# The last eight blocks of an expert layer in nested branches, with a change of w2 and the last down product taken by halves

## What is computed

```python
def _moe2_ref(x, modality_id, w_gate, modality_bias, w1, w2):
    N, D = x.shape                      # 3072 tokens, 384; 8 experts; w1: 384 x 1024, w2: 1024 x 384 each
    logits = x @ w_gate + modality_bias[modality_id]
    e_idx = np.argmax(logits, axis=1)
    ...
    gate_w = probs[np.arange(N), e_idx]
    for e in range(E):
        mask = e_idx == e
        if not mask.any():
            continue
        h = np.maximum(x[mask] @ w1[e], 0.0)
        out[mask] = gate_w[mask, None] * (h @ w2[e])
```

## Time and profile before

| | us |
|---|---|
| median of 3 runs | 916.67 (913.45 to 918.15) |
| the profiled execution | 912.8 |
| its span, first to last instruction | 911.1 |
| PE busy with matmuls | 835.3 (92% of the span) |
| mean granted clock of TensorE | 0.968 |

### The profile page before, as it was taken

The page is one execution under the profiler, slowest core; times in us unless marked ns, Lnnn a source line. Parts: engine busy times, 40 slices in busy tenths (PEclk is TensorE's granted clock), DMA queues, the critical chain, the costliest instruction groups (busy, mean ns, idle before and its releaser), DMA issues.

```text
span 911.1 us, 26166 instructions
## 1 busy us (share of the span) xinstructions
PE 835.3 (92%) x10528; PEld 740.3 (81%) x10529; DVE 567.3 (62%) x1598; ACT 351.0 (39%) x613; POOL 86.4 (9%) x100
## 2 busy tenths in 40 slices
PE   3674699999999999999999999999989999999993
PEld 3564588889888888888888888789868999999993
DVE  5958896888677877787688843344743333333342
ACT  4463246443644454345533432424412222222231
POOL 1000000000010000100010000010121222212211
PEclk9977699999999999999999999999999999999997
DMA  8942453256226541484134313246151111111104
GB/s 120 306 110 46 85 136 80 65 110 135 48 55 111 119 72 29 101 147 72 29 90 99 71 44 80 56 85 204 35 174 45 43 44 35 51 36 43 43 19 148
DMA packets 148679, 77.94 MB, mean 86 GB/s; under 512 B 112864, under 2 KB 144608, under 8 KB 148192
## 3 DMA queue, kind: packets, MB, share of 16 engines
q1 hardware_dynamic: 143632, 66.59, 33.1%
q0 software_dynamic: 4096, 9.48, 3.4%
q10 hardware_dynamic: 848, 0.39, 0.2%
HBM read 59.30 MB, written 13.21 MB: 80 GB/s over the span
## 4 chain that ended last, share of the span: by engine, by line
PE 79%; DVE 5%; ACT 5%; DMA 3%; SPq 3%; issue 3%; ACTq 1%; POOL 0%; DVEq 0%; POOLq 0%
PE bank L560 21%; PE bank L541 19%; PE bank L627 11%; PE bank L652 10%; PE bank L637 2%; ACT gram_d L1081 2%; PE bank L442 2%; PE bank L462 2%; PE bank L411 1%; PE bank L522 1%; PE bank L490 1%; PE bank L422 1%; PE bank L473 1%; PE bank L398 1%; DMA kq_in_rows<-in_k 1%
## 5 line engine op out<-in xcount | busy, mean ns | idle before, releaser
L560 PE MATMUL bank<-wo_hi,g_hi 128*128 128x392 f32 x384 | 135.6, 353 | 1.9 <-DVE g_lo L1536 1.9
L560 PE MATMUL bank<-wo_lo,g_hi 128*128 128x392 f32 x384 | 131.1, 341 | 0.0
L560 PE MATMUL bank<-wo_hi,g_lo 128*128 128x392 f32 x384 | 130.8, 341 | 0.0
L541 PE MATMUL bank<-x_hi,wi_hi 128*128 128x512 f32 x288 | 119.9, 416 | 11.3 <-DVE x_lo L1527 10.6
L1154 ACT ACTIVATE g_raw<-bank 128x512 f32<-128x512 f32 x96 | 57.4, 598 | 169.6 <-PE bank L541 169.4
L1531 DVE SCALAR_TENSOR_TENSOR g_raw<-g_raw 128x512 f32<-128x512 f32 x96 | 66.1, 688 | 81.8 <-ACT g_raw L1154 81.2
L541 PE MATMUL bank<-x_hi,wi_lo 128*128 128x512 f32 x288 | 114.5, 397 | 0.0
L541 PE MATMUL bank<-x_lo,wi_hi 128*128 128x512 f32 x288 | 114.4, 397 | 0.0
L1161 ACT ACTIVATE g_hi<-g_raw 128x512 fp32r<-128x512 f32 x96 | 60.8, 633 | 98.9 <-DVE g_raw L1531 98.9
L1536 DVE TENSOR_TENSOR g_lo<-g_raw,g_hi 128x512 fp32r<-128x512 f32 x96 | 66.1, 689 | 30.9 <-ACT g_hi L1161 29.6
L560 PEld LDWEIGHTS bank<-wo_hi,g_hi 128*128 128x128 f32 x384 | 72.3, 188 | 7.1 <-issue 3.1
(11 more groups left out here) (215 smaller groups left out, 1451.3 us busy)
## 6 DMA issues: line engine op xcount, KB each, us to landing
wo_lo<-wo_lo_d SPq DMA_DIRECT2D x80, 196.0 KB, 2.6
w_raw<-in_moe_w SPq DMA_DIRECT2D x4, 1536.0 KB, 7.8
x_rows<-stage SPq DMA_DIRECT2D x24, 192.5 KB
kq_in_rows<-in_k SPq DMA_DIRECT2D x6, 768.0 KB, 7.0
k_raw<-in_k SPq DMA_DIRECT2D x24, 192.0 KB, 4.1
vals<-in_v SPq DMA_DIRECT2D x48, 96.0 KB, 2.7
kq_in_rows<-in_q SPq DMA_DIRECT2D x6, 768.0 KB, 7.0
x_raw<-y_t SPq DMA_DIRECT2D x33, 96.0 KB, 2.5
```

What stands on the lines that cost most here:

```text
L541: mm = pe.matmul(bank[0][:], a[:, m, P * f:P * f + P], x[:, m, :], start=(m == 0 and x is x_hi and a is wi_hi), stop=(m == KT - 1 and a is ...
L560: mm = pe.matmul(acc[i][:, 0:DX], g[f % 2][:, P * i:P * i + P], w, start=(f == 0 and k == 0), stop=(f == FT - 1 and k == 2))
```

## The change

Three things are changed.

1. Blocks 23 to 30 are written out, each in the branch of the block before, with no loop. Their table loads have fixed addresses. When block 25 has no tokens, one jump leads behind all of it.
2. In `act_block` and `dve_block`, for all blocks from 2 on, the second half of a new w2 is made behind `split_ht`, and on DVE behind `gated` too, not ahead of them. The decision is loaded once and branched on twice.
3. The down product that comes by itself behind the last block waits by halves: for the first half of `w_lo` and `ht_lo`, then 12 matmuls, then for the second half, then 12 matmuls.

```diff
-            def block_down(x, count=None):
+            def block_down(x, count=None, by_halves=False):
...
-                pe.wait_ge(w2l[0], count)
-                pe.wait_ge(w2l[1], count)
-                pe.wait_ge(s.ht_rdy, b * 2 + 2)
+                if not by_halves:
+                    pe.wait_ge(w2l[0], count)
+                    pe.wait_ge(w2l[1], count)
+                    pe.wait_ge(s.ht_rdy, b * 2 + 2)
                 for h in range(2):
+                    if by_halves:
+                        pe.wait_ge(w2l[h], count)
+                        pe.wait_ge(s.ht_rdy, b * 2 + h + 1)
...
-            with pe.Fori((TOKT - 1) // 2, (BLOCKS - 1) // 2) as i:
-                with pe.If(has_tokens(pe, Blk(i, 1)) > 0):
-                    pe_block(Blk(i, 1))
-                    with pe.If(first_without(pe, Blk(i, 2)) > 0):
-                        block_down(Blk(i, 1))
-                    with pe.If(has_tokens(pe, Blk(i, 2)) > 0):
-                        pe_block(Blk(i, 2))
-                        with pe.If(first_without(pe, Blk(i, 3)) > 0):
-                            block_down(Blk(i, 2))
+            def last_blocks(x):
+                pe_block(x)
+                with pe.If(first_without(pe, x.next()) > 0):
+                    block_down(x, by_halves=True)
+                if x.n < BLOCKS - 1:
+                    with pe.If(has_tokens(pe, x.next()) > 0):
+                        last_blocks(x.next())
+
+            last_blocks(Blk(0, TOKT - 1))
...
             def act_block(x):
...
-                with act.If(changes(act, x) > 0):
-                    change_w2(x)
+                change = changes(act, x)
+                with act.If(change > 0):
+                    change_w2(x, 0)
                 split_ht(x.n)
+                with act.If(change > 0):
+                    change_w2(x, 1)
...
             def dve_block(x, kept=False):
...
-                with dve.If(changes(dve, x) > 0):
-                    change_w2(x)
+                change = changes(dve, x)
+                with dve.If(change > 0):
+                    split_w2(0, expert_count(dve, x))
                 gated(x.next(-1))
                 split_ht(x.n)
+                with dve.If(change > 0):
+                    split_w2(1, expert_count(dve, x))
```

## The result

| | us |
|---|---|
| before, median of 7 runs | 913.76 (912.04 to 918.15) |
| changed, median of 7 runs | 909.73 (907.89 to 910.92) |
| ratio changed to before | 0.9935, 95% interval 0.9919 to 0.9951 |
| profiled execution of the changed kernel | 909.23, its span 907.4 |

The ratio is 5.9 us of 913.76 (4.5 to 7.4). The difference of the two medians is 4.0 us and that of the two means 5.2, so the size of the gain is uncertain by some 1.5 us. I had forecast 3.1. The direction was right and the size was not; the time lies nearest to rival (a). It is 3.9 us under the 913.6 that I named, but 2.9 of that is the kernel of before, whose median came out at 913.76 here and at 916.67 in the three runs that I added my forecast to. So the gain is what is to be compared, and not the time.

What follows compares the result with a forecast made beforehand. It took the kernel to be bound by PE's matmuls (79% of the span). With `o_sb` 3.7 us earlier but the drain starting at the landing, it gained 3.1 us: 916.67 - 3.1 = 913.6 us, range 909.0 to 918.5.

Steps and rivals of the forecast that it cites:

- rival (a): At the end, POOL's drain runs beside the transfers: gain 5.7 us, 911.0, or 912.4 with the lower clock; chance 0.32.
- The chain in block 24: Last down product: PE's gap shrinks from 4.2 to 1.9 us, a 0.25 us wait inside, `o_sb` 3.7 us earlier.
- The clock: PE's clock stays at its upper level in the last down product, giving 1.4 of the 3.7 us.
- The empty turns: At the end, POOL's three empty loop turns go, so its drain is reached at most 2.0 us earlier.
- The landing: Block 24's scatter, started at 897.9, lands at 901.5, just behind the load of w2.
- The drain: At the end, POOL's 6.3 us drain starts only when the last scatter lands: end at 908.0, gain 3.1 us.
- (b): Last scatter held up by the load, taking 7.4 us to land: 917.4 us; chance 0.18 together with smaller losses.
- (c): At the end, the jump over six blocks costs POOL 2.1 us of code fetch: 913.1 us; chance 0.07.
- (d): Blocks 3 to 22: one more branch on ACT and DVE holds up the sequencer: slower, 923.6 us; chance 0.05.

Runs made afterwards that it cites:

- e6: The changed kernel, with POOL waiting until its last scatter has landed before it goes to the drain; ratio to before 0.9975.
- e0: The kernel of before, unchanged, profiled once more in one execution; 912.54 us.
- e3: The changed kernel, with its last down product waiting for everything at once as before; ratio to before 0.9988.
- e2: The kernel of before with its loop, with w2 and ht by halves and the last down product waiting by halves; ratio to before 0.9955.
- e7: The changed kernel without the scatter of block 24 and without the unused loads behind the last expert; ratio to before 0.9860.
- e5: The changed kernel without the unused loads of w1 and w2 behind the last expert; ratio to before 0.9917, 908.11 us.

## Why the prediction was right and wrong, step by step

**The chain in block 24: right.** I said a gap of 1.9 us, a stop of 0.25 in the middle, and `o_sb` 3.7 us earlier from the last turning; measured 1.70, 0.16 (0.05 ahead of the 13th matmul and 0.11 behind it) and 3.84. **The clock: right, by a choice that no row settled.** It stayed at 1.00 throughout; ahead of the last product it fell with gaps of 3.7 to 4.3 us in every profile, and with 1.7 to 1.8 in none. In between it goes either way: behind block 4's gather PE stood for 2.4 to 2.6 us, and the clock fell to 0.50 in the changed kernel and 0.54 in e6, but not in e0 and e3. It also fell behind the broken stretch of the earlier trace rows, so a short gap alone is no guarantee.

**The empty turns: right in kind, 1.5 us and not 2.0.** I let the drain begin at the end of the scatter instruction, with 6.3 us; it takes 6.3 to 6.45 us from there, a little more than the 6.28 of a POOL that comes late.

**The landing: 0.7 us short, and without consequence.** I put it at 901.5 for a scatter started at 897.9, 3.6 us; it took 4.3. It did come when I said, just behind the load of w2 (903.7 and 903.5).

**The drain: wrong, and this step carries nearly the whole error.** "I take the first reading of the drain, by a little ... no row decides it." The sum let the 6.3 us begin at the landing, 901.5, and not at 898.9, where POOL is through with its scatter; those 2.6 us were never spent. The trace held one fact, that 6.28 us passed with the scatter landed, and both readings fit it. The changed kernel, e2 and e6 decide for the other one: the drain is over 3.1 us behind the landing, takes its 6277 ns with the scatter in flight, and waiting for the landing first adds the wait in full (13.0 us behind `o_sb`, not 9.5). By rival (a) the sum was 5.7 us; the profiles show 5.4 and the runs 5.9 (the profiles' sum is 3.8 from the chain, where I had 3.7, and 1.5 from the turns, where I had 2.0). The Trainium skill, page "VectorE: DVE Perf Modes", section "The DRAIN you can't avoid", puts the drains that the runtime adds at a program's beginning and end at a constant of about 12 ns on all engines. The drain here stands in the kernel's own closing barrier, and the traces don't tell whether the section would count it; POOL's is 6.19 to 6.94 us in eleven profiles, and the measurement decides.

**The rivals.** (a) came true, at the upper clock. (b), a late landing, could not matter. (c), the fetched code, is real as a stall (that it is a fetch is argued only), and mostly larger than I priced it (2.6 to 6.6 us against 2.1), but falls on the engines that POOL covers, and not on POOL. (d), the extra branch in blocks 3 to 22, costs nothing. The turning of h in block 3 and that in block 24 stand 21 blocks apart; the first of them in the changed kernel:

```profile
691.11 1.03 PE L637 MATMUL bank<-ident,h_sb 128*128 128x128 f32 x8
```

From there to 890.59 it is 199.5 us; in the kernel of before the same stretch ran from 689.16 to 888.93, 199.8 us.

**The chances.** I gave no clear change 0.57 and faster by over 0.5% only 0.36, and it came out faster by 0.65%. The two readings of the drain lay on either side of that bound, and I had leaned to the wrong one.

## What to carry over

Read the end of a program backwards from its last instruction: here 6.3 of the 22 us behind the last block's turning were the drain of one engine, and 2.0 more its empty turns ahead of it, so what counts is when that engine is through with its last transfer instruction and at its drain. When halves are taken in turn, move both sides at once: the producer's order without the consumer's wait, or the wait without the order, gained nothing at `o_sb`. And when one measured duration allows two readings that price a change differently by 2.6 us, the forecast is as uncertain as the choice between them.

## What the runs showed of the hardware that I had not expected

- POOL's drain in the closing barrier ended 6.2 to 6.45 us behind the end of its last indirect transfer's instruction, or behind POOL's arrival where that was later, landed or not, and with the last transfer left out too. POOL's 2.0 us of empty turns before it took nothing off (6.28 us in before, e0 and e2).
- A taken branch over the code of six blocks held PE's sequencer for 3.3 and 3.6 us without weight loads (e7, e5) and for 5.4 to 6.6 us beside one; over the loop body of before it took 0.21 us.
- After a stand of 2.4 to 2.6 us, PE was granted the lower clock in two profiles and the upper in two others.
- The last scatter took 2.1 to 4.7 us to land, from kernel to kernel, and 3.5 in e5, with no weight load beside it.
